# A scan at the end of the slot in front, an earlier first product, and two row copies on ScalarE's queue

## The reference, cut to what matters

```python
mag = np.sqrt(a_re * a_re + a_im * a_im)
scale = np.minimum(mag, 0.999) / (mag + 1e-06)
a_re_n, a_im_n = (a_re * scale, a_im * scale)
for t in range(S):
    ar, ai = (a_re_n[:, :, t, :, None], a_im_n[:, :, t, :, None])
    new_re = ar * S_re - ai * S_im
    new_im = ar * S_im + ai * S_re
    kv = np.einsum('bhd,bhe->bhde', k[:, :, t], v[:, :, t])
    S_re, S_im = (new_re + kv, new_im)
    y[:, :, t] = np.einsum('bhd,bhde->bhe', q[:, :, t], S_re)
# layer 1: h = x @ w_in; g = h * clip(h + 3, 0, 6) / 6; x = g @ w_out
# layer 2: h = x @ w_in; g = max(h, 0) + alpha * min(h, 0); out = g @ w_out
```

## Time and profile before

| | us |
|---|---|
| median of 3 runs | 1030.25 (1028.29 to 1031.63) |
| the profiled execution's own time | 1026.65 |
| its span | 1024.7 |
| PE busy in the span | 967.1 (94%) |
| DVE, ACT, POOL busy | 599.4, 485.4, 263.2 |
| mean granted TensorE clock | 0.986 of full |

### The profile page before, as it was taken

One profiled execution on the slowest core, in us unless ns is written; L12 is line 12 of the kernel. 1 busy time (PEld: TensorE's weight loads), 2 busy tenths in 40 slices (PEclk: granted clock), 3 DMA queues, 4 the chain that ended last, 5 costly groups with the idle time before them and its releaser, 6 DMA issues.

```text
span 1024.7 us, 17083 instructions
## 1 busy us (share of the span) xinstructions
PE 967.1 (94%) x6498; PEld 869.2 (85%) x6498; DVE 599.4 (58%) x1088; ACT 485.4 (47%) x865; POOL 263.2 (26%) x235
## 2 busy tenths in 40 slices
PE   0799987999999999999999999999999999999997
PEld 0788877899999999999999998888888888888886
DVE  6767787778878878878772244453433433434332
ACT  7656666667677676777743453221221222212211
POOL 0000022222222222322222243333333333323332
PEclk9999988999999999999999999999999999999999
DMA  6752322333433333442221611001010010100000
GB/s 171 207 141 70 86 70 71 87 85 95 106 82 94 85 94 77 104 110 71 78 68 27 241 61 54 1 20 43 1 62 1 1 62 1 62 1 1 32 1 31
DMA packets 80930, 70.48 MB, mean 69 GB/s; under 512 B 32592, under 2 KB 78160, under 8 KB 80464
## 3 DMA queue, kind: packets, MB, share of 16 engines
q1 hardware_dynamic: 80208, 68.80, 24.7%
q10 hardware_dynamic: 640, 0.59, 0.3%
HBM read 40.90 MB, written 9.44 MB: 49 GB/s over the span
## 4 chain that ended last, share of the span: by engine, by line
PE 83%; SPq 5%; ACT 4%; DVE 4%; DMA 2%; issue 2%; DVEq 0%; ACTq 0%
PE op L1189 12%; PE op L1190 12%; PE hp L1190 12%; PE op L1191 12%; PE hp L1189 12%; PE hp L1191 11%; SPq L402 3%; PE yp L1177 3%; PE gp L1156 3%; SPq L405 2%; PE yp L1156 2%; DMA st<-prod 2%; PE gp L1184 2%; PE hp L1212 1%; PE tp L1165 1%
## 5 line engine op out<-in xcount | busy, mean ns | idle before, releaser
L524 POOL TENSOR_TENSOR g_lo<-gated,g_hi 128x384 fp32r<-128x384 f32 (+2 forms) x224 | 261.0, 1165 | 752.1 <-ACT g_hi L620 752.1
L620 ACT ACTIVATE g_hi<-gated 128x384 fp32r<-128x384 f32 (+2 forms) x224 | 123.3, 551 | 330.0 <-DVE gated L904 284.4
L900 DVE TENSOR_SCALAR gate<-hp,alpha_sb 128x512 f32<-128x512 f32 x96 | 72.1, 751 | 240.0 <-PE hp L1191 240.0
L889 DVE SCALAR_TENSOR_TENSOR gated<-gate,hp 128x384 f32<-128x384 f32 (+1 forms) x144 | 72.8, 506 | 125.3 <-ACT gate L613 125.0
L1189 PE MATMUL op<-g_hi,wb_hi 128*128 128x384 f32 (+1 forms) x384 | 129.3, 337 | 0.4 <-ACT out_sb L625 0.2
L1189 PE MATMUL hp<-x_hi,wa_hi 128*128 128x384 f32 (+1 forms) x384 | 126.0, 328 | 0.0
L613 ACT ACTIVATE gate<-hp,half 128x384 f32<-128x384 f32 (+1 forms) x144 | 77.2, 536 | 101.9 <-PE hp L1191 87.7
L1191 PE MATMUL op<-g_hi,wb_lo 128*128 128x384 f32 (+1 forms) x384 | 124.8, 325 | 0.0
L1190 PE MATMUL op<-g_lo,wb_hi 128*128 128x384 f32 (+1 forms) x384 | 124.7, 325 | 0.0
L1191 PE MATMUL hp<-x_hi,wa_lo 128*128 128x384 f32 (+1 forms) x384 | 123.7, 322 | 0.0
L1190 PE MATMUL hp<-x_lo,wa_hi 128*128 128x384 f32 (+1 forms) x384 | 123.6, 322 | 0.0
(11 more groups left out here) (110 smaller groups left out, 1704.1 us busy)
## 6 DMA issues: line engine op xcount, KB each, us to landing
st<-prod SPq DMA_DIRECT2D x92, 145.1 KB, 2.9
a_sb<-a_in SPq DMA_DIRECT2D x24, 288.0 KB, 4.0
qk_sb<-qk_in SPq DMA_DIRECT2D x24, 288.0 KB, 3.6
v_pad<-v_in SPq DMA_DIRECT2D x24, 192.0 KB, 3.8
x_raw<-x SPq DMA_DIRECT2D x6, 768.0 KB, 5.6
out<-out_sb SPq DMA_DIRECT2D x6, 768.0 KB, 4.0
st<-prod SPq DMA_DIRECT2D x96, 32.2 KB, 2.3
wa_raw<-w_in SPq DMA_DIRECT2D x6, 512.0 KB, 6.1
```

What stands on the lines that cost most here:

```text
L524: pool.tensor_tensor(g_lo[:, at, 0:wide], gated[:, at * UT:at * UT + wide], g_hi[:, at, 0:wide].bitcast(F32), ALU.subtract).then_inc(glo_d ...
L620: act.activation(g_hi[:, at, 0:wide], gated[:, at * UT:at * UT + wide], ACT.Copy).then_inc(ghi_done, 1)
L889: dve.scalar_tensor_tensor(out=gated[:, to], in0=gate[:, at], scalar=1.0, in1=hp[:, n % 2, 0:wide], op0=ALU.min, op1=ALU.mult).then_inc(ga ...
L900: dve.tensor_scalar(gate[:, at], hp[:, n % 2, 0:wide], 0.0, alpha_sb[:, m:m + 1], ALU.min, ALU.mult).then_inc(gate_done, 1)
```

## The change

The plans and lengths of the slots are new; the scan `forward` of the chunk two ahead stands at the end of the slot in front; ACT's small copy into `prod` goes from `b` to `c`, its squares from `j` to `o`; in slots of short units (and for chunk 2) two of the twelve row copies go from SP's queue to ACT's.

```diff
-SHORT = {6: ("a", "bf", "cdo", "egv", "hij", "kl"), 7: ("a", "bf", "cdo", "egv", "hi", "j", "kl")}
-LONG = {5: ("ab", "cdefg", "ov", "hij", "kl"), 6: ("ab", "cdefg", "ov", "hij", "kl", "")}
+SHORT = {6: ("a", "cf", "deo", "glv", "hij", "kb"), 7: ("a", "cf", "deo", "glv", "hi", "j", "kb")}
+LONG = {5: ("a", "cdefg", "ov", "hij", "klb"), 6: ("a", "cdefg", "ov", "hij", "klb", "")}
-LENGTHS = (6, 6, 6, 6, 7, 7, 7) + 4 * (5, 5, 6) + (5, 6, 6)
+LENGTHS = (7, 7, 7, 6, 6, 6, 6) + 4 * (5, 5, 6) + (5, 6, 6)
+def is_short(s):
+
+    return width(items_of(s)[-1] // MT_FF) == FIRST * CH
+
+
+def two_queues(c):
+
+    return c <= FIRST or is_short(c - 1)
...
@@ SP, stack(c)
-                for to, rows in high_stack(c, 1) + ([] if c < FIRST else low_stack(c, 1)):
+                for to, rows in high_stack(c, 1) + ([] if two_queues(c) else low_stack(c, 1)):
                     sp.dma_start(to, rows).then_inc(st_landed[c % 2], 16)
...
@@ ACT, before and in the loop over places()
             inverses(3)
+            stack(2)
             gate_of(0)
...
+                if "o" in steps and c3 is not None:
+                    squares(c3)
                 if "v" in steps and c2 is not None:
                     inverses(c2)
                 if "h" in steps:
                     x_high(c0)
-                if "j" in steps and c3 is not None:
-                    squares(c3)
+                    if c1 is not None and two_queues(c1):
+                        stack(c1)
                 if "k" in steps and c2 is not None:
                     angle(c2)
                 if n + GSTEP >= MT_FF:
                     high(n + GSTEP)
-                if "b" in steps and c1 is not None:
+                if "c" in steps and c1 is not None:
                     copy_ends(c1)
...
@@ DVE, before and in the loop over places()
             mags(4)
+            forward(3)
             gate1(3)
...
                 if "a" in steps and c1 is not None:
                     phases(c1)
                     fractions(c1)
-                    if "b" in steps:
-                        forward(c1)
                 gate1(n + GSTEP)
-                if "b" in steps and "a" not in steps and c1 is not None:
-                    forward(c1)
                 if "c" in steps and c1 is not None:
                     backward(c1)
...
                 if "l" in steps and c3 is not None:
                     mags(c3)
+                if "b" in steps and c2 is not None:
+                    forward(c2)
```

More of the change, by code:

```diff
@@ L126, in places @@
         items = items_of(s)
-        plan = (SHORT if width(items[-1] // MT_FF) == FIRST * CH else LONG)[len(items)]
+        plan = (SHORT if is_short(s) else LONG)[len(items)]
         for steps, n in zip(plan, items):
```

## The result

The changed kernel takes 1023.4 us (median of 5 runs, 1019.2 to 1023.85) against 1030.25 (5 runs, 1027.48 to 1031.63): a ratio of 0.993, with an interval of 0.9904 to 0.9957. So the change gains 7 us. The forecast was 1012, from 1003 to 1023: the sign was right, the gain was 0.4 of what was expected, and the median lies 0.4 us above the range. The profiled execution took 1022.65 us, 4.0 less than the one of before, with a span of 1020.9.

The account below looks back on a forecast made before the run. PE's waits for row copies in short slots, with the clock dips behind them, cost 30 us at most. Slots gain 18.9, long slots give back 0.7: net 18.2, profiled 1026.65 to 1008.4, median 1012.0, range 1003 to 1023.

Parts of the forecast that it names:

- the copies' chain: Short slots, first row copy to next scores: two copies on ACT's queue make it 8.0 us, not 9.7 to 10.3.
- Rival 2: Slots of chunks 4 to 8: split copies land no sooner; 10.3 us worse than forecast, 1022; chance 0.20.
- the two new waits: `hidden(16)` and `hidden(48)` wait for `x_low` of chunks 3 and 8: 0.4 us each, bounded by 0 and 1.5.
- the signs that were named: Short stage if right: clock 1.00 but in chunk 6's slot, chunk 8's first copy 11.5 us in, chunk 9's scores at 218.
- one sign of being wrong: Slots of chunks 4 and 5: PE waits for masks or low parts of g beyond 2 us.
- Forward at the slot's end: DVE, end of each slot: no work added, fractions delayed some 1.4 us, covered until the next slot's second gate.
- the long slots: The 14 long slots: 0.5 us later by slot, costing 0.7 us where copy slack is less; bounds 0 and 5.
- Rival 3: Long slots: copies start later through `copy_ends` and later fractions, slack is lost, ending near 1036; chance 0.05.
- chunk 2's slot: First short slot, seven items: 24.3 us with copies landing before its end, ending at 86.6.
- the later start: Before the loop: ACT's two new issues for chunk 2 ahead of `gate_of(0)` cost 0, at most 1.25 us.
- chunks 4, 5, 7 and 8: Short slots forecast at 22.1, 23.5, 19.5 and 20.5 us.
- The doubt about a backlog: Chunk 5's slot: DVE arrives with a backlog, first product ends 15.5 us in, slot takes 23.5 us.

Follow-up runs that it names:

- a5: Changed kernel with all twelve row copies on SP's queue again from chunk 2 on: 1025.56 us, ratio 0.9975 to the kernel before.
- b1: Kernel before with only the second queue added, two row copies on ACT's queue for chunks 3 to 9: 1015.91 us, ratio 0.9862.
- a1: Changed kernel with chunk 2's twelve copies all on SP's queue again: 1021.82 us, ratio 0.9936 to the kernel before.
- a2: Changed kernel with `forward` moved from the end of the slot in front to the next slot's first item, behind gate1: 1015.48 us, ratio 0.9875.
- a4: Changed kernel with the long slots' plan and order as before the change, short slots staying changed: 1018.77 us, ratio 0.991.
- b0: Kernel before, unchanged, run again for a second profile: 1028.91 us, ratio 1.0015.
- a7: Changed kernel with the slot lengths of before, (6, 6, 6, 6, 7, 7, 7): 1020.01 us, ratio 0.992 to the kernel before.
- a6: Changed kernel with `forward` behind the first item's gate1 and ACT's logs in the third item of short slots: 1015.89 us, ratio 0.9871.
- a3: Changed kernel with ACT's logs an item later, in the third item of short slots: 1022.75 us, ratio 0.9935 to the kernel before.
- a9: Changed kernel with `forward` behind the first gate, the old slot lengths, and the long slots in the order of before: ratio 0.9831.
- a8: Changed kernel with `forward` behind the first gate and the slot lengths of before: 1010.79 us, ratio 0.9815 to the kernel before.
- b2: Kernel before with the new slot lengths alone, (7, 7, 7, 6, 6, 6, 6): 1034.29 us, ratio 1.0039.

## Why the prediction was right or wrong

**Right, the copies' chain.** In chunk 7's slot SP's first copy starts at 198.85 and the scores at 206.77, 7.9 us; in chunk 8's slot at 221.00 and 229.11, 8.1 us; in those of chunks 4 to 6 it takes 8.0 to 8.5. The forecast was 8.0 against 10.3. SP issues six and then four:

```profile
198.85 3.84 SPq L413 DMA_DIRECT2D st<-prod  x6
202.74 2.69 SPq L416 DMA_DIRECT2D st<-prod  x4
```

ACT's two, at 202.42 and 203.04, come 16.6 and 17.2 us into the slot; 14.8 + 0.9 = 15.7 was the estimate for the first of them. Rival 2 falls for these slots, and a5 and b1 put 4.6 and 14 us on the second queue. The rule of the Trainium skill that was weighed there ("DMA: Bandwidth & Descriptors", "Issuing engines are not separate DMA queues") holds at the start, where the engines are full (share 1.14) and a1 shows no gain from the second issuer, and its "usually small" doesn't hold for twelve issues of 0.65 us in a row.

**Right, the two new waits.** `hidden(16)` and `hidden(48)` wait 0.24 and 0.46 us for `x_low`; 0.4 each was said.

**Of the signs that were named,** these failed: the clock, which was to be 1.00 but in chunk 6's slot, is 0.90, 0.93, 0.92 and 0.92 in those of chunks 2, 5, 6 and 7; the first copy of chunk 8's slot starts 14.2 us in, not 11.5; chunk 9's scores start at 229.11, not 218. And one sign of being wrong came: in the slots of chunks 4 and 5 PE waits 2.5 us for masks and low parts of g, and 2.9 more for gated values.

**Wrong, the step "*Forward at the slot's end.* No DVE work is added ... cover is the time until the next slot's second gate".** It was costed at nothing. The wait for copies was itself that cover. In chunk 8's slot of before the fractions end 2.4 us in, and DVE waits 2.39 us for the gate at 218.64:

```profile
215.36 0.56 DVE L800 TENSOR_TENSOR t_frac<-t_phase,t_trig 128x384 f32<-128x384 f32 x1
```

The change takes that wait away, so DVE comes into the slot with `lost` and `decays` undone and then a scan ahead of the phases. The fractions end 5.7 us in, the waves wait, the second gate comes 2.8 us later into the slot, and the product ends 14.1 us in, not 11.5. Of these 2.6 us a2 gives 1.5 back; the other 1.1 go, as far as the timelines tell, with DVE's late arrival, which a2 shares. In chunk 5's slot the product ends 17.1 us in where 15.5 was said, and a2 gives 1.3 back.

Not every late slot is bound so. In chunk 7's slot the fractions end 2.3 us in, and the second gate waits for PE:

```profile
192.01 0.47 ACT L624 ACTIVATE gate<-hp,half 128x256 f32<-128x256 f32 x1 [1.41 <-PE hp L1204]
```

PE runs there at a clock of 0.92, behind a wait of 2.17 us for copies; the product ends 12.9 us in, 1.4 late. That is a dip which the forecast had in chunk 6's slot alone. In a2 a wait of 2.03 us stands there, the clock stays at 1.00 and the slot takes 19.3 us, as forecast; that so small a difference decided it may be luck.

**Wrong, the long slots.** Forecast 0.7, with bounds of 0 and 5; it came to 3.7, and a2 gives back 3.2 of it, a4 3.5. The reckoning looked at slacks of the copies; what was short of slack was, by the waits, the mask in front of `outputs`. Rival 3 had the stage and the later fractions right, but put the loss on the start of the copies.

**Wrong, chunk 2's slot.** 24.3 us was said, 26.9 came, with PE busy all the time at a clock of 0.90. PE stood ready at 60.4 and waited 3.88 us for copies, where in the profiled execution of before it came at 62.2 and did not wait. Its first scores then took 2.08 us in place of 1.16. The copies land late because the engines are full. How long PE waits there differs between executions of one kernel: 0 in the profile of before, 3.16 us in b0. Over the other profiles it goes from 1.66 to 5.05 us. The clock of the slot follows it only loosely: 1.00 behind 1.66 to 2.68 us (a7, a6, b1, a3) and behind 3.16 (b0), 0.90 to 0.93 behind 3.88 and more (the change, a1, a4, a9, a8, a5), but 0.88 behind 2.01 (b2) and 3.13 (a2).

The 2 us later start is another matter. The four profiles of kernels that start as before (before, b0, b1, b2) have chunk 2's scores at 62.2 to 63.1, the ten that start as the changed kernel, or nearly, at 63.6 to 65.3, without an overlap. So the later start does seem to come with the change, and the forecast had it at nothing, at most 1.25. Taking out ACT's two issues alone (a1, a5) or the forward scan of the start alone (a2, a6, a8, a9) doesn't give it back, and no run takes out both: which edit costs it stays open.

**Mis-sized, chunks 4, 5, 7 and 8.** They took 1.5, 1.7, 1.5 and 1.8 us more than forecast. In chunk 5's slot PE also waits for DVE directly, 2.64 us for a gated value at 146.45. The doubt about a backlog was right in kind, and its size was too small, since it wasn't confined to that slot. There is also a slip of 0.2 us in the reckoning of a late slot: from 10.8 for the product's start, with half of 1.82 us for its first half, the end is 11.7, not 11.5. Sum of the seven slots: 155.5 forecast, 164.9 measured, and this 9.4 with 3.0 for the long slots and 2.0 for the start makes the 14 us between the forecast of 1008.4 and the profiled 1022.65. The scan's place (a2) gives back 4.9 of it in the slots of chunks 3 to 8 and 3.2 in the long ones; 4.6 lie in the start and in chunk 2's slot, and some 2 stay open.

**The parts don't add up.** The second queue alone gives 14 us, the new lengths alone take 4, and the whole gives 7. The forecast put 18.9 on one picture in which each part helps the next. My reading, which a2 supports and no run isolates: a short wait for copies is where DVE and ACT recover, so a second edit on the same wait finds less to take, and one that makes DVE later costs where before it was free.

## What to carry to other kernels

Before removing a wait, ask which other queues used it to catch up: work that was costed at nothing because of that wait has a price afterwards. Work that the next gate doesn't need belongs behind the gate, where its engine would wait anyway. And time the parts of a bundled change alone: here one part was worth twice the whole.

## What the runs showed of the hardware

A DVE scan can take more than twice its time where it meets a low part of g on POOL, but only in one position. In the changed kernel the three forward scans at 208.40 take 1.55 us, where the earlier trace rows have 1.05: the first and the last take 0.4 us each and the middle one 0.90. In a2 the phases' three at 204.75 take 1.67, where the changed kernel's at 210.29 take 1.23. POOL's timeline of the changed kernel, then a2's:

```profile
208.47 0.89 POOL L535 TENSOR_TENSOR g_lo<-gated,g_hi 128x256 fp32r<-128x256 f32 x1 [3.10 <-ACT g_hi L631]
```

```profile
204.94 0.83 POOL L535 TENSOR_TENSOR g_lo<-gated,g_hi 128x256 fp32r<-128x256 f32 x1 [3.10 <-ACT g_hi L631]
```

The slow scan at 208.74 begins inside POOL's instruction and ends 0.3 us behind it. Counted over the scans of all fourteen traces: none of the 2200 that meet no POOL instruction takes over 0.49 us, nor does any of the 308 during which POOL's instruction begins, and the 101 wholly inside one take 0.40 each; of the 415 that begin inside one and outlast it, 278 take over 0.6 us, up to 1.25. In the long stage 19 scans of the changed kernel are slow, 13 of them forward scans, against 15 in the kernel of before. So where a scan stands against POOL's work is part of its price. No run took one of the two away, so the cause is argued from these positions alone.

A wait doesn't settle the clock by its length alone. Ahead of chunk 2, waits of 2.68 us (a3) and 3.16 us (b0) left the slot at 1.00, while 2.01 us (b2) and 3.13 us (a2) stand ahead of slots at 0.88; in the changed kernel 2.38 and 2.17 us stand ahead of slots at 0.92.
